# Fused attention and two MLP blocks in float32: moving the first down weights' low part and one input's low part from VectorE to GpSimd

## What is computed

```python
# attention: a window of 15 neighbours each side, and 24 block summaries (max of k, mean of v) per head
x = softmax(masked local scores and summary scores) @ [v, v_sum]      # (2, 768, 512) after the heads are joined
# block 1: mixing over tokens, then over channels
h = relu(x^T @ w_tok1) @ w_tok2
u = x + h^T
x = u + relu(u @ w_ch1) @ w_ch2                                        # 512 -> 1536 -> 512
# block 2
xn = (x - mean) / sqrt(var + 1e-6) * g_ln
out = x + relu(xn @ w2_ch1) @ w2_ch2                                   # 512 -> 2048 -> 512
```

## Time and profile before

| | us |
|---|---|
| median of 3 runs | 588.18 |
| lowest, highest | 587.4, 588.22 |
| the profiled execution, its own time | 587.95 |
| its span in the trace | 586.2 |
| TensorE (PE) busy | 572.7 |
| VectorE (DVE) busy | 300.1 |
| ScalarE (ACT) busy | 229.0 |
| GpSimd (POOL) busy | 227.7 |

### The profile page before, as it was taken

How to read it: one execution, slowest core, us unless ns; L and a number is a source line. 1 busy time by engine, 2 the same in 40 slices (tenths; PEclk the granted TensorE clock), 3 DMA queues, 4 the chain that set the end, 5 groups by cost and what they waited for, 6 DMA issues and landing times.

```text
span 586.2 us, 8260 instructions
## 1 busy us (share of the span) xinstructions
PE 572.7 (98%) x2976; PEld 500.1 (85%) x2976; DVE 300.1 (51%) x653; ACT 229.0 (39%) x432; POOL 227.7 (39%) x225
## 2 busy tenths in 40 slices
PE   6799999998999999999999999999999999999997
PEld 2687888887889988998888899988989888989896
DVE  6376556497444345753445665443334644444444
ACT  3377664571333334263235333633435222121210
POOL 4477665317344466020317974543468000000000
PEclk9799999999999999999999999999999999999999
DMA  8878731074544374444413374544374333443602
GB/s 234 242 202 240 200 110 33 1 258 173 198 158 143 118 303 165 156 161 162 162 37 115 119 251 169 187 183 166 159 286 163 143 129 128 145 151 148 234 0 108
DMA packets 26912, 94.38 MB, mean 161 GB/s; under 512 B 7820, under 2 KB 8056, under 8 KB 23288
## 3 DMA queue, kind: packets, MB, share of 16 engines
q1 hardware_dynamic: 26320, 93.41, 46.4%
q10 hardware_dynamic: 552, 0.44, 0.3%
HBM read 64.42 MB, written 28.84 MB: 159 GB/s over the span
## 4 chain that ended last, share of the span: by engine, by line
PE 91%; DMA 2%; POOL 2%; DVE 2%; ACT 1%; issue 1%; SPq 1%; POOLq 0%; ACTq 0%
PE bank L594 87%; PE bank L697 1%; DMA k_sb<-k_w 1%; POOL v_tree L441 1%; PE bank L627 1%; PE bank L629 1%; PE bank L628 1%; DMA v_far<-v_mean 1%; DMA v_turned<-v_t 1%; PE bank L688 0%; DVE natural L1115 0%; ACT in_t L923 0%; POOL x_split L455 0%; DVE in_t L1065 0%; DVE k_sb L1071 0%
## 5 line engine op out<-in xcount | busy, mean ns | idle before, releaser
L594 PE MATMUL bank<-down_w,hidden 128*128 128x512 f32 x1008 | 270.0, 396 | 1.3 <-DVE natural L1115 1.3
L594 PEld LDWEIGHTS bank<-down_w,hidden 128*128 128x128 f32 x1008 | 184.5, 188 | 26.6 <-issue 1.6
L960 ACT ACTIVATE hidden<-bank 128x384 fp32r<-128x384 f32 x112 | 55.1, 492 | 249.5 <-DVE bank L1144 179.8
L594 PE MATMUL bank<-in_t,up_even 128*128 128x384 f32 x588 | 119.1, 337 | 0.6 <-DVE hidden L1136 0.6
L594 PE MATMUL bank<-in_t,up_odd 128*128 128x384 f32 x588 | 118.8, 336 | 0.0
L594 PEld LDWEIGHTS bank<-in_t,up_even 128*128 128x128 f32 x588 | 105.2, 188 | 10.6 <-DVE hidden L1136 1.4
L594 PEld LDWEIGHTS bank<-in_t,up_odd 128*128 128x128 f32 x588 | 105.6, 188 | 9.0
L1136 DVE SCALAR_TENSOR_TENSOR hidden<-bank,hidden 128x384 fp32r<-128x384 f32 x112 | 62.5, 558 | 86.6 <-ACT hidden L960 86.6
L1176 DVE TENSOR_TENSOR u<-bank,p 128x384 f32<-128x384 f32 x28 | 15.6, 558 | 89.3 <-PE bank L594 89.3
L1144 DVE TENSOR_TENSOR bank<-bank,u 128x384 f32<-128x384 f32 x84 | 47.5, 565 | 20.4 <-PE bank L594 15.8
L1083 DVE CUSTOM_DVE_ANT_0 neg_scores<-bank,mask_sb 128x182 f32<-128x182 f32 x96 | 29.5, 344 | 29.5 <-PE bank L594 26.6
(11 more groups left out here) (94 smaller groups left out, 604.0 us busy)
## 6 DMA issues: line engine op xcount, KB each, us to landing
raw_down<-w_ch SPq DMA_DIRECT2D x28, 512.0 KB, 3.3
up_kept<-up_even SPq DMA_DIRECT2D x7, 1792.0 KB, 8.1
up_kept<-up_odd SPq DMA_DIRECT2D x7, 1792.0 KB, 8.1
up_even<-up_kept SPq DMA_DIRECT2D x7, 1792.0 KB, 7.6
up_odd<-up_kept SPq DMA_DIRECT2D x7, 1792.0 KB, 7.0
raw_up<-w_ch SPq DMA_DIRECT2D x14, 512.0 KB, 4.2
k_sb<-k_w SPq DMA_DIRECT2D x16, 273.0 KB, 4.5
v_own<-v_w SPq DMA_DIRECT2D x8, 390.0 KB, 3.3
```

The source lines that it names most:

```text
L594: return nc.tensor.matmul(dst, lhs, rhs, start=start, stop=stop, skip_group_check=True)
L960: nc.scalar.activation(hidden[:, q % 2, f, 0, h * HN:(h + 1) * HN], src, ACT.Relu).then_inc(hid_high, 1)
```

## The change

Three edits, all of them about pair 0, and the waits that go with them. The low part of pair 0's down weights is made on GpSimd (`first_low_down`), behind `low_first(1)` of VectorE; its high part moves forward on ScalarE, ahead of `high_input(0, 1)`. The low part of input 5 is made on GpSimd, where that of input 6 follows it, both ahead of `low_up(1)`. On VectorE `sum_first(3)` moves behind `add_mixed(1, 0)`, and `add_mixed(1, 1)` and `add_mixed(1, 2)` each move one place back. The down products wait for `u_done` at token tiles 2 and 3 only.

```diff
@@ SyncE, load_down
-                    sp.wait_ge(down_low, q - 1)
+                    wait_down_low(sp, q - 2)
@@ GpSimd
             def low_first(i):
                 pool.wait_ge(in_high, i + 1)
-                nc.gpsimd.tensor_tensor(in_t[:, i, 1], raw_block(i), in_t[:, i, 0].bitcast(F32), ALU.subtract
+                src = t_in[:, T_OF[i]] if i in T_OF else raw_block(i)
+                nc.gpsimd.tensor_tensor(in_t[:, i, 1], src, in_t[:, i, 0].bitcast(F32), ALU.subtract
                                         ).then_inc(first_low_pool, 1)
+                pool.wait_ge(first_low_pool, i - 4)
+
+            def first_low_down():
+                pool.wait_ge(down_high, 1)
+                pool.wait_ge(in_low, 2)
+                nc.gpsimd.tensor_tensor(down_w[:, 0, :, 1, :], raw_down[:, 0], down_w[:, 0, :, 0, :].bitcast(F32),
+                                        ALU.subtract).then_inc(down_low_pool, 1)
+                pool.wait_ge(down_low_pool, 1)
...
+            first_low_down()
             for q in range(NQ):
                 g, j = group_of(q)
                 making = q + 1 < NQ and is_made(q + 1)
+                if q == 0:
+                    pool.wait_ge(in_low, 5)
+                    low_first(5)
+                    low_first(6)
...
                 if making:
                     low_up(q + 1)
-                if q == 0:
-                    low_first(6)
-                if making and j < PAIRS_OF[g] - 1:
-                    pool.wait_ge(down_low, q + 1)
+                if making and q and j < PAIRS_OF[g] - 1:
+                    wait_down_low(pool, q)
@@ TensorE, up
-                if q == 0 and i < 6:
+                if q == 0 and i < 5:
                     pe.wait_ge(in_low, i + 1)
                 elif q == 0:
-                    pe.wait_ge(first_low_pool, 1)
+                    pe.wait_ge(first_low_pool, i - 4)
@@ TensorE, down
                 if (t, f) == (0, 0):
-                    pe.wait_ge(down_low, q + 1)
+                    wait_down_low(pe, q)
                     pe.wait_ge(hid_low, 4 * q + 3)
-                    if q == 0:
-                        pe.wait_ge(u_done, 2 * NT)
+                if q == 0 and t in (2, 3) and f == 0:
+                    pe.wait_ge(u_done, NT + t + 3)
@@ ScalarE, pair
                 if q == 0:
                     high_input(0, 4)
-                    high_down(0)
-                    high_input(0, 5)
...
                 high_hidden(q, 0, product_bank(q, 2)[:, 0:HN])
                 if q == 0:
+                    high_input(0, 5)
                     high_input(0, 6)
@@ ScalarE, ahead of the pairs
             high_input(0, 0)
+            high_down(0)
             high_input(0, 1)
@@ VectorE, pair
                     add_mixed(1, 0, o_bank[0])
+                    sum_first(3, blk(1, 0), t_in[:, 1])
                     low_first(4)
...
                 low_hidden(q, 0, product_bank(q, 2)[:, 0:HN])
-                if q == 0:
-                    add_mixed(1, 1, o_bank[1])
-                    low_first(5)
...
                 if q == 0:
-                    add_mixed(1, 2, o_bank[0])
+                    add_mixed(1, 1, o_bank[1])
...
+                if q == 0:
+                    add_mixed(1, 2, o_bank[0])
                 low_hidden(q, 1, product_bank(q, 4)[:, 0:HN])
@@ VectorE, ahead of the pairs
             low_first(2)
             low_first(3)
-            sum_first(3, blk(1, 0), t_in[:, 1])
-            low_down(0)
```

More of the change, by code:

```diff
@@ L218, in build @@
         down_low = sem("down_low")
+        down_low_pool = sem("down_low_pool")
         nat_ready = sem("nat_ready")
@@ L253, in build, with wait_down_low @@
         up_kept = nc.dram_tensor("up_kept", [NMADE, P, 2 * 7 * 2 * P], F32, kind="Internal").ap()
+        def wait_down_low(engine, q):
+            if q:
+                engine.wait_ge(down_low, q)
+            else:
+                engine.wait_ge(down_low_pool, 1)
         def wait_downs(engine, q):
@@ L896, in copy_batch @@
                 if i == 0 and g == 1:
-                    act.wait_ge(in_low, 6)
-                    act.wait_ge(first_low_pool, 1)
+                    act.wait_ge(in_low, 5)
+                    act.wait_ge(first_low_pool, 2)
                 if i == 0 and g > 1:
```

## The result

| | before | after |
|---|---|---|
| median of 7 runs, us | 587.4 | 583.72 |
| lowest, highest, us | 586.28, 588.57 | 583.06, 584.87 |
| profiled execution, us | 587.95 | 583.59 |
| its span, us | 586.2 | 581.8 |

The ratio is 0.9939, 95% interval 0.9926 to 0.9952: faster, by 2.8 to 4.3 us. The kernel before now has seven runs, the three of the table ahead of the prediction among them.

A forecast was written before the change was run, and what follows sets the result against it. TensorE was taken as busy nearly everywhere, so only closing its gaps pays: 3.05 us lost around pair 0, less 0.1 for one meeting, gives 2.95 off the median 588.18, so 585.2 us, range 584.4 to 586.8.

The forecast's parts named there:

- The gap: TensorE from 124.05 to 144.40 us: 20.35 us holding 17.30 us of work, so 3.05 us lost to waits and restarts.
- the sum: Whole kernel: 3.05 less 0.1 gives 2.95 us gained, taken from the median of 588.18 to forecast 585.2 us.
- Part 1: Down weights' low part leaves VectorE for GpSimd: `u2` starts 1.4 us sooner, one meeting stalls TensorE 0.1 us.
- Part 2: Down weights' high part moves forward on ScalarE: costs nothing, with 0.4 us of cover from VectorE's queue.
- Parts 3 and 4: VectorE's new order and GpSimd's input 5 in pair 0: products 3 to 6 start unstalled at 129.9, 132.3, 134.7, 137.1.
- part 4: Input 5 on GpSimd: ready at 133.0, wanted at 134.7; nothing meets, and a later load keeps over 5 us to spare.
- The tight place: `add_mixed(1, 2)` ahead of the fifth mixing group in pair 0: a wait of nothing to 0.2 us, taken as 0.
- Part 5: The first down product no longer waits for the last `add_mixed`: the 1.33 us gap of TensorE goes.
- the half case: Rival in pair 0: three worse bounds and restarts return part of the gain, 1.7 us remain, 586.4 us; chance 0.10.
- a new wait in pair 1: Rival: GpSimd and SyncE run 4.9 us later against TensorE, pair 2's weights come late, time 588; no change given 0.07.
- The late load: Rival: pair 0's down weights landing beyond 4.1 us hold ScalarE, one us lost per us, 590.1 at 9 us; chance 0.03.

The follow-up runs named there:

- experiment 5: The changed kernel with the down weights' low part back on VectorE, behind `low_first(3)`: 584.82 us, ratio 0.9949 against the kernel before.
- experiments 9 and 10: The changed kernel with pair 0's down weights loaded behind one other load, then behind two: 585.93 us, ratio 0.9965; and 588.93 us, ratio 1.0011.
- experiment 7: The kernel before with one edit, GpSimd waiting for `low_first(5)` of VectorE ahead of `low_up(1)`: 586.49 us, ratio 0.9979.
- experiment 6: The changed kernel with input 5's low part back on VectorE, behind `add_mixed(1, 1)`: 584.77 us, ratio 0.9947 against the kernel before.

## Why the prediction was right, and where it failed

**The gap.** Predicted: of 3.05 us that can be had, 2.95. Measured in the stretch: 2.98, 3.00 and 2.99 us in three executions against 20.35. The upper bound was sized a little short: 3.09 were had in experiment 5, since the 0.76 us of the down unit held 0.06 of restart (it takes 139.33 to 140.03, 0.70, in the changed kernel), which the sum counted as work.

**Part 1.** The meeting came as worked out: GpSimd began 0.1 us behind the start of pair 0, ran 2.41 us, `low_first(2)` was held to its end, and TensorE lost 0.11 us for the 0.1 taken. `u2` was predicted 4.05 us behind the start of pair 0 and came at 126.77 - 122.66 = 4.11. But I read part 1 as a gain ("1.4 us sooner") without asking who still needed it. Experiment 5 shows that nobody did, once `sum_first(3)` and the cast had moved: product 3 wants `u2` later than VectorE has it with the down weights in front. Of the 1.4 us, 1.05 came there without GpSimd, and part 1 put them all under the move to it.

**Part 2.** Cover of 0.4 us, price nothing: right. The cast waited for its data (0.42 us idle) and TensorE saw nothing of it. What it costs if the cover is gone was put at one us per us beyond 4.1, and experiments 9 and 10 measured 1.00. By that rule the two lose 1.4 and 3.7 us; they lost 1.26 and 3.56.

**Parts 3 and 4.** Products 3 to 6 were predicted at 129.9, 132.3, 134.7 and 137.1, that is 5.9, 8.3, 10.7 and 13.1 us behind the start; they came 5.98, 8.39, 10.81 and 13.22 behind it. GpSimd's input 5 started 7.16 us behind it, predicted 7.1 (its end at 133.0 less 1.85); no row met another. One reading in part 4 was too wide: it set the start of `sum_weights(3)` past 153.4 from the row of 151.01, and left out that this row moves with the gain. In the changed kernel it stands at 146.63, 4.4 us sooner in the span (3.0 of it the gain, 1.4 the start), so the slack was 3 us smaller than the "over 5" put down; GpSimd did not wait for that load all the same. The tight place held (VectorE's `natural` row at 133.43 ends at 134.11, the group started at 134.51), and experiment 6 shows how near it was: there VectorE came to its sum behind product 4 some 0.85 us later against the start of pair 0, and 0.63 us of that reached the stretch.

**Part 5.** The 1.33 us gap went, as predicted; but its worth depends on the company it is in: 1.34 us alone, 0.44 with the rest.

**What the sum left out.** Its parts were priced from the rows that surround them, and it did not say which of them would do alone. Two edits of one place each give most of the gain: VectorE and GpSimd no longer hold each other off inside pair 0 (1.71 us alone), and the down products wait for fewer adds (1.34 alone), 2.65 together. The changed kernel gets rid of the meetings by another way than experiment 7, by its order and the wait for `in_low` 5; that its gain splits in the same way is argued from that and not measured.

**The step that failed** is not in the 2.95 us but in what they were taken from: the last line of the sum, "against the median: 585.2 us", and with it the low end, "584.4 (the full 3.05 us, and 0.7 since the lowest run shown lies 0.78 under the median)". It took the median of three runs as the kernel's level and their spread as its scatter. With seven runs the median before is 587.4, and 587.4 to 587.9 in the later comparisons: 588.18 was 0.8 too high, and 2.95 off 587.4 is 584.45. That is 0.73 above the measured 583.72. This remaining 0.7 lies ahead of pair 0, in a term that the sum put at nothing without a reason: one trace shows one start of pair 0, and I took it as fixed, where the traces have 122.3 to 127.9. The likely gain of 2.95 us is a ratio of 0.9950 and lies inside the intervals of all three comparisons of the changed kernel (0.9926 to 0.9952, 0.9913 to 0.9955, 0.9905 to 0.9955), near their upper ends. The three medians are 3.7, 3.4 and 3.7 us apart from those of before. The 0.4 to 0.7 us beyond the stretch are an earlier start of pair 0 (123.2 for 123.8 in the medians above). Its cause stays open: it came in all three comparisons of the changed kernel, but not in the kernels that differ from it only inside pair 0 or in the burst of loads.

**The rivals.** Neither the half case nor a new wait in pair 1 came: what follows the stretch is 441.8 us in both. The half case also counts the stall of product 2 twice, as 0.1 and again within 0.85, which changes its 1.7 us by 0.1. The late load is real as a mechanism and didn't occur.

## What to carry to other kernels

When several waits follow each other on one path, price each fix alone and again with the others in place: here the move of the down weights' low part looked like the core of the change and was worth nothing beside the rest, while one added wait on an engine with time to spare, which kept two engines from holding each other off, was worth 1.7 us. Read a gain from the stretch that the change touches, where it repeats within 0.02 us; the level of the whole run, and so the bounds of a forecast in us, needs many executions and an allowance for stages that the change doesn't touch.

## What the runs showed of the hardware

Two subtractions with all operands in SBUF, one on VectorE and one on GpSimd, ran one after the other in every meeting that the rows here show in and ahead of pair 0, whichever came first: 0.95 us became 2.10, 1.77 and 2.12 on VectorE, 1.85 became 2.42 and 2.44 on GpSimd. What I had not expected is how much this is worth to a third engine: more than half of TensorE's loss in pair 0 (1.71 of 3.05 us). Over the whole span VectorE is only 51% busy, but in the 20.35 us of the stretch before the change it was busy for 17.20 us, the time it was held included, so there a hold has little slack to hide in.

Nor had I expected the end of attention to move by 5.6 us between executions of the same TensorE instructions, with the granted clock falling only in its first 45 us, while what follows the stretch took 441.73 to 441.87 us in all 14 traces.
